# Tables by GpSimd, odd inverse decays through PSUM, earlier rows and scatter of each third chunk, and W2's first load moved to the fourth half

## The reference

```
state = 0
for t in range(768):                                   # per batch and head
    y[t]  = r[t] @ (state + outer(u * k[t], v[t]))
    state = w[t][:, None] * state + outer(k[t], v[t])
x = y as 3072 tokens x 384
h = x @ w_in;  g = max(h, 0) + alpha * min(h, 0);  x = g @ w_out       # 384 -> 2048 -> 384
expert = argmax(x @ w_gate);  gate = softmax(x @ w_gate)[expert]       # 8 experts
out = gate * (max(x @ w1[expert], 0) @ w2[expert])                     # 384 -> 1024 -> 384
```

## Time and profile before

| | us |
|---|---|
| median of 3 runs | 778.72 (777.6 to 780.84) |
| profiled execution, its own time | 781.25 |
| its span | 779.5 |
| PE busy | 733.1 (94%) |
| DVE, ACT, POOL busy | 475.7, 365.6, 392.9 |
| first output product of g = 0, 1, 2, 3, 4, 5, 6, 7 | 50.6, 122.8, 184.2, 248.4, 309.4, 370.8, 432.2, 491.0 |

### The profile page before, as it was taken

How to read it: one execution, slowest core, us unless ns; L and a number is a source line. 1 busy time by engine, 2 the same in 40 slices (tenths; PEclk the granted TensorE clock), 3 DMA queues, 4 the chain that set the end, 5 groups by cost and what they waited for, 6 DMA issues and landing times.

```text
span 779.5 us, 17757 instructions
## 1 busy us (share of the span) xinstructions
PE 733.1 (94%) x6779; PEld 516.6 (66%) x6779; DVE 475.7 (61%) x967; ACT 365.6 (47%) x735; POOL 392.9 (50%) x372
## 2 busy tenths in 40 slices
PE   4699999999989999999999999998999999999995
PEld 4466656656655665665666666556688878788783
DVE  6998898779666878776787864645333333333331
ACT  3652577656655756746756665542122212212210
POOL 5445488769668869778777876252111111111111
PEclk9998999999999999999999999999999999999998
DMA  9835636365364653645545247994699866766763
GB/s 341 324 150 185 209 132 244 105 241 174 131 238 179 234 215 121 233 165 172 201 142 187 82 162 243 341 345 158 225 383 395 294 245 214 254 237 219 265 222 116
DMA packets 42694, 170.04 MB, mean 218 GB/s; under 512 B 5198, under 2 KB 13136, under 8 KB 37104
## 3 DMA queue, kind: packets, MB, share of 16 engines
q1 hardware_dynamic: 30160, 108.18, 39.1%
q10 hardware_dynamic: 8928, 50.51, 18.5%
q0 software_dynamic: 3520, 10.17, 3.3%
HBM read 132.30 MB, written 37.33 MB: 218 GB/s over the span
## 4 chain that ended last, share of the span: by engine, by line
PE 60%; POOL 9%; DMA 9%; DVE 6%; issue 6%; ACT 3%; SPq 1%; ACTq 0%; POOLq 0%; DVEq 0%
PE bank L1733 5%; PE bank L1876 5%; PE bank L1878 5%; PE bank L1877 5%; PE bank L1735 4%; PE bank L1734 4%; PE bank L1724 4%; PE bank L1722 4%; PE bank L1721 4%; PE bank L1842 4%; PE bank L1844 4%; PE bank L1843 4%; DMA arena<-w_exp_dram 3%; POOL act_buf L606 3%; DMA route_rows<-xrow,pos 2%
## 5 line engine op out<-in xcount | busy, mean ns | idle before, releaser
L606 POOL TENSOR_TENSOR act_buf<-act_buf 128x384 f16<-128x384 f32 x128 | 120.2, 939 | 139.8 <-ACT act_buf L809 138.8
L1291 DVE SCALAR_TENSOR_TENSOR act_buf<-neg,slope,bank 128x384 f32<-128x384 f32 x128 | 77.7, 607 | 92.1 <-ACT neg L802 91.4
L692 POOL DMA_INDIRECT out_dram<-neg,dest x28 | 27.5, 984 | 201.7 <-DVE neg L1560 194.2
L1733 PE MATMUL bank<-arena,act_buf 128*128 128x392 f16 x384 | 127.2, 331 | 1.6 <-ACT xrow L765 1.4
L1721 PE MATMUL bank<-xh,arena 128*128 128x384 f16 x384 | 125.5, 327 | 2.2 <-DVE xl L1093 1.5
L1734 PE MATMUL bank<-arena,act_buf 128*128 128x392 f16 x384 | 127.1, 331 | 0.0
L1735 PE MATMUL bank<-arena,act_buf 128*128 128x392 f16 x384 | 127.0, 331 | 0.0
L1722 PE MATMUL bank<-xl,arena 128*128 128x384 f16 x384 | 125.3, 327 | 0.0
L1842 PE MATMUL bank<-shared,arena 128*128 128x128 f16 x672 | 114.1, 219 | 1.9 <-DVE shared L1486 1.7
L1844 PE MATMUL bank<-shared,arena 128*128 128x128 f16 x672 | 114.1, 219 | 0.0
L1843 PE MATMUL bank<-shared,arena 128*128 128x128 f16 x672 | 114.1, 219 | 0.0
(11 more groups left out here) (185 smaller groups left out, 1563.9 us busy)
## 6 DMA issues: line engine op xcount, KB each, us to landing
arena<-expert_split ACTq DMA_DIRECT2D x28, 1536.0 KB, 7.5
arena<-w_exp_dram SPq DMA_DIRECT2D x32, 768.0 KB, 6.3
expert_split<-arena SPq DMA_DIRECT2D x32, 768.0 KB, 4.7
arena<-expert_split SPq DMA_DIRECT2D x9, 1536.0 KB, 9.2
arena<-rk_in_dram SPq DMA_DIRECT2D x24, 512.0 KB, 6.0
arena<-rk_tok_dram SPq DMA_DIRECT2D x24, 384.0 KB, 3.3
arena<-w_dram SPq DMA_DIRECT2D x24, 256.0 KB, 6.8
shared<-route_rows ACTq DMA_DIRECT2D x31, 197.0 KB, 2.5
```

The lines of the kernel that those rows point to most:

```text
L606: pool.tensor_tensor(gl[:, f % 4, :], gf[:, f % 4, :], gh[:, f % 4, :], ALU.subtract).then_inc(gl_done, 1)
L1733: pe.matmul(at, gh[:, f % 4, ts], woh[:, f, :], start=(f == 0), stop=False)
```

## The change

Seven of the eight small table copies go from DVE's turn 13 of g = 0 to POOL's start; the eighth, of an unused tensor, goes. Where the hidden bank of the turn is free, the reciprocals are written there, multiplied from there, and copied to their place (`inverses_through`), for chunk 2 in turn 1 and chunk 1 in turn 14 of g > 0; hidden tiles 2 and 4 wait for that. `y_rows` of chunk 2 goes from turn 13, behind the product of tile 13, to turn 12. The scatters go ahead of the decayed k and q of their turn, the third from turn 15 to 14. `load_w2(0)` is issued in the middle of SP's list of g = 3.

```diff
 # SP, middle(g, j)
                 if b < B:
                     load_tok(b, half, 1)
                     load_v(b, half, 1)
+                if g == 3:
+                    sp.wait_ge(wide_free[0], 4)
+                    load_w2(0)
                 store_hu(j + 1)
                 load_hu(j + 3)
...
             for g in range(1, 2 * B - 1):
                 middle(g, FIRST_UNIT[g] // 2)
-                if g == 2:
-                    sp.wait_ge(wide_free[0], 4)
-                    load_w2(0)
 # POOL
+            pool.wait_ge(pool_const, 3)
+            pool.tensor_copy(expert_no[:, :], iota_i[:, 0:NE])
+            pool.tensor_copy(token_no[:, :], iota_i[:, 8:8 + NC])
+            pool.tensor_copy(region[:, :], iota_i[:, 16:16 + NE])
+            pool.tensor_copy(slot_no[:, :], iota_i[:, 32:32 + REST])
+            pool.tensor_copy(begin[:, :], iota_i[:, 16:16 + NE + 1])
+            pool.tensor_copy(lane[:, :], iota_i[:, 8:9])
+            pool.tensor_copy(next_row[:, :], iota_i[:, 16:16 + NE + 1]).then_inc(pool_const, 1)
...
                         if f in lows and not end:
                             unit_low(unit + lows.index(f))
+                        if not start and not end and f in (12, 13, 14):
+                            scatter(g - 1, f - 12)
                         if not last:
                             if f == 11:
                                 decayed_k(b + 1, half, 0)
...
-                        if not start and not end and f in (12, 13, 15):
-                            scatter(g - 1, (12, 13, 15).index(f))
 # DVE
+            def inverses_through(b, half, c, odd, read):
+                m, at = 6 * b + 3 * half + c, (half + c) % 2
+                dve.wait_ge(scan_done, m + 1)
+                dve.wait_ge(kt_done, m - 1)
+                dve.wait_ge(g_done, UP + read)
+                dve.reciprocal(odd.rearrange("p (a j) -> p a j", a=NP),
+                               prod[:, c, :, 1:C + 1].rearrange("p a (j r) -> p a j r", r=2)[:, :, :, 1]
+                               ).then_inc(odd_done, 1)
+                dve.wait_ge(odd_done, m + 1)
+                every_second = inv[:, at, :].rearrange("p (j r) -> p j r", r=2)
+                dve.tensor_tensor(every_second[:, :, 0], odd,
+                                  w_tile(m).rearrange("p (j r) -> p j r", r=2)[:, :, 1], ALU.mult)
+                dve.tensor_copy(every_second[:, :, 1], odd).then_inc(inv_done, 1)
...
                         if not start and f == 1:
-                            inverses(nb, nh, 2)
+                            inverses_through(nb, nh, 2, b_hid[f][:, 0:NP * C // 2], NF * g + f + 1)
...
                         if f % 4 == 1 and f > 3:
                             if update(nh, c) and nh + c > 0:
                                 decayed_state(nb, nh, c)
-                            y_rows(nb, nh, c, b_y)
+                            if f < 13:
+                                y_rows(nb, nh, c, b_y)
...
                         if f == 12:
                             decays(b + 1, half, 1, b_hid[f][:, 0:C])
+                    if not end and f == 12:
+                        y_rows(nb, nh, 2, b_y)
...
-                    if start and f == 13:
-                        dve.wait_ge(pool_const, 3)
-                        dve.tensor_copy(ident_h[:, :], ident[:, :])
-                        dve.tensor_copy(expert_no[:, :], iota_i[:, 0:NE])
-                        dve.tensor_copy(token_no[:, :], iota_i[:, 8:8 + NC])
-                        dve.tensor_copy(region[:, :], iota_i[:, 16:16 + NE])
-                        dve.tensor_copy(slot_no[:, :], iota_i[:, 32:32 + REST])
-                        dve.tensor_copy(begin[:, :], iota_i[:, 16:16 + NE + 1])
-                        dve.tensor_copy(lane[:, :], iota_i[:, 8:9])
-                        dve.tensor_copy(next_row[:, :], iota_i[:, 16:16 + NE + 1]).then_inc(dve_const, 1)
                     if not last:
-                        if f == 14:
+                        if f == 14 and start:
                             inverses(b + 1, half, 1)
+                        if f == 14 and not start:
+                            inverses_through(b + 1, half, 1, b_hid[f][:, 0:NP * C // 2], NF * g + f + 1)
 # PE, hidden(...)
+                if f == 2 and not first and not last_half:
+                    pe.wait_ge(inv_done, NC * (g + 1) + 2)
+                if f == 4 and not first and not last_half:
+                    pe.wait_ge(inv_done, NC * (g + 1) + 3)
```

More of the change, by code:

```diff
@@ L90, in build @@
         ident = sb("ident", [128, 128], F32)
-        ident_h = sb("ident_h", [128, 128], F16)
         earlier = sb("earlier", [128, C], I32)
@@ L458, in _, with load_w2 @@
             load_tok(1, 0, 2)
+            def load_w2(e):
+                for i in range(2):
+                    sp.wait_ge(split_out[i], UP + 16 * (2 * e + 2))
+                sp.dma_start(arena[:, w2_at(e):w2_at(e) + 2 * UNIT], wsplit[e][:, 2 * UNIT:4 * UNIT]
+                             ).then_inc(w2_in[e], 16)
             def middle(g, j):
@@ L1301, in mlp @@
                         if not start and f == 1:
-                            inverses(nb, nh, 2)
+                            inverses_through(nb, nh, 2, b_hid[f][:, 0:NP * C // 2],
+                                             NF * g + f + 1)
                         if f == 2:
@@ L1350, in mlp @@
                         w_out_low(1, f // 11)
-                    if start and f == 13:
-                        dve.wait_ge(pool_const, 3)
-                        dve.tensor_copy(ident_h[:, :], ident[:, :])
-                        dve.tensor_copy(expert_no[:, :], iota_i[:, 0:NE])
-                        dve.tensor_copy(token_no[:, :], iota_i[:, 8:8 + NC])
-                        dve.tensor_copy(region[:, :], iota_i[:, 16:16 + NE])
-                        dve.tensor_copy(slot_no[:, :], iota_i[:, 32:32 + REST])
-                        dve.tensor_copy(begin[:, :], iota_i[:, 16:16 + NE + 1])
-                        dve.tensor_copy(lane[:, :], iota_i[:, 8:9])
-                        dve.tensor_copy(next_row[:, :], iota_i[:, 16:16 + NE + 1]).then_inc(dve_const, 1)
                     if not last:
-                        if f == 14:
+                        if f == 14 and start:
                             inverses(b + 1, half, 1)
+                        if f == 14 and not start:
+                            inverses_through(b + 1, half, 1, b_hid[f][:, 0:NP * C // 2],
+                                             NF * g + f + 1)
                         if f == 15:
@@ L1366, in mlp @@
                     if start and f == 15:
-                        dve.wait_ge(dve_const, 3)
+                        dve.wait_ge(pool_const, 4)
                     if not start and not end:
```

## The result

The changed kernel is slower: 796.54 us median of 6 runs (791.18 to 801.52) against 776.53 for the kernel before (its three runs and three more), a ratio of 1.0252 (95% interval 1.0216 to 1.0287). The forecast was 773.0.

The account below looks back on a forecast made before the run. TensorE, busy 733.1 of 779.5 us, was taken as the bound, so only earlier starts count. Gains 5.2 + 2.5 + 0 + 0 - 2.0 = 5.7 us took the median 778.72 to 773.0, range 768.0 to 778.0.

Parts of the forecast that it names:

- Odd inverses in PSUM: Turns 1 and 14: multiply and copy take 0.84 us against 0.42 to 3.32; worth nothing, 1 us lost as other end.
- the chain above: VectorE's queue from `row_sums` of turn 15 through `v_low` to `att_l`: 1.2 us given back in g=2, 0.2 in g=4.
- the one above it: The step on tables made by POOL, which quoted a multiply with two SBUF inputs taking 0.42 us once and 3.32 elsewhere.
- Third scatter: Scatter in turn 14: ScalarE's row copy waits only for PE; row copy and `att_l` waits go, 2.5 us gained, bounds 1.5 and 2.5.
- Third y rows: `y_rows` in turn 12 ahead of product 13: 6.6 us of `ytok` waits and clock gained, 1.4 given back, net 5.2.
- The four waits: PE's waits for `ytok` in g=1, 2, 4 and 5 (1.06, 2.09, 1.19, 0.54 us), forecast to go.
- the 1.7 of clock: 1.7 us lost in g=2 to PE's lower clock level after the idle 2.09 us, counted as regained.
- W2's load: In g=3 it delays the unit conversion of turn 12 (wait about 7.6 us for 3.68); PE idles 2.0, bounds 0 and 9.
- Tables: Small copies moved from VectorE in g=0 to POOL's start: PE then waits for a DMA-bound scan; nothing, 0.4 lost to 1.6 gained.
- The waits for the inverses: PE's hidden products of tiles 2 and 4 wait for inverses made over 3 and over 1 us earlier; cost nothing.
- Rival B: POOL and VectorE behind the late unit are the bound; 1 us more given back in five halves: 777.5; chance 0.15.
- C: W2 in the full stretch of g=3 decides: 780.0 us, over 782.6 if other loads are late too; chance 0.06.

Follow-up runs that it names:

- run 1: Changed kernel with the inverse of turn 1 made in SBUF without the copy, as before: 777.84 us against 777.35, ratio 1.0001.
- run 4: Changed kernel with one wait added on POOL: the decayed k of chunk 2 in turn 1 waits for `v_low` of chunk 0: 771.86 us, ratio 0.9942.
- run 2: Kernel before with only the inverse of turn 1 through PSUM, hidden tile 4 waiting for it: 778.33 us against 777.35, ratio 1.0012.
- run 5: Kernel before with only the scatters moved (turns 12, 13, 14, ahead of the decayed q): 774.30 us against 775.59, ratio 0.9975.
- run 6: Kernel before with the scatters moved and the inverse of turn 1 through PSUM: 787.77 us, ratio 1.0168.
- run 10: Kernel before with `y_rows` of the third chunk in turn 12 and the scatters moved, every inverse in SBUF: 773.06 us, ratio 0.9965.
- run 12: Kernel before with only the tables made by POOL at the start: 776.40 us against 775.61, ratio 1.0005.
- run 8: Changed kernel with POOL's decayed k of chunk 2 waiting for `v_low` and W2's load back behind the list of g=2: 768.55 us, ratio 0.9909.
- run 3: Changed kernel with `v_low` of chunk 0 moved from turn 2 to turn 3: 791.59 us, ratio 1.0165.
- run 13: Changed kernel with a write-only POOL memset added in turn 1 before the decayed k of chunk 2: 801.39 us against 776.22, ratio 1.0321.
- run 14: Changed kernel with a POOL copy from SBUF to SBUF added in turn 1 before the decayed k of chunk 2: 801.24 us, ratio 1.0316.
- run 15: Changed kernel with W2's load behind the list of g=2 as before: 785.57 us, ratio 1.0105.

## Why the prediction was wrong

- **The step that failed** is that of *Odd inverses in PSUM*: "it is already in the chain above, and where PE doesn't wait for that chain it is worth nothing". The chain had `v_low` in it as one more item, at the lengths of before (0.55 to 1.37 in the trace), although the same step and the one above it quoted 3.32 for another instruction with two SBUF operands. The slow multiply of turn 1 was not only a cost. POOL's decayed k waits for it by semaphore, so POOL stood for some 0.4 us in most halves; the multiply got through there, and `v_low` behind the instruction that followed. Made fast, it let POOL run on, and `v_low` took over its place with a longer hold: 5.8 for 3.3. PE then waited 15.7 us for `att_l` and lost 6.0 to the clock, where the step said nothing, or 1 us at its other end. Runs 1 and 4 take the loss away from the changed kernel, runs 2, 5 and 6 build it up in the kernel before.
- *Third scatter*: right in its size alone (774.30 for 775.59; 2.5 us taken, 1.9 by the ratio). What it did besides was the second half of the loss: it removed the other pause, POOL's wait for ScalarE.
- *Third y rows*: 5.2 us taken, nothing alone and about 0.8 beyond the scatters (0.9965 for 0.9975, the intervals overlap). The four waits went as I said; the loss at the boundary was mis-sized. I had the chain to `att_l` and left the row copy out of this step, because another part of the change was to mend it: 3.23 us and its clock. Beside the scatters the row copy is no longer late, and still little is left: against run 5, run 10 waits 3.3 us less for `ytok`, 1.9 more for `att_l` and 1.6 more for the hidden product behind VectorE's. And the 1.7 of clock came from one profile; runs 5 and 12 have `ytok` as before, their longest waits for it are 1.5 us, and no lower level follows.
- *W2's load*: right in mechanism, mis-sized in time. ScalarE's wait in turn 12 of g=3 came to 8.09 us in the changed kernel against my 7.6. PE paid 1.08 and 0.80 us there, near my 2.0, if by luck in part: the wait at the next boundary, in which I had put most of it, can't be told from the hold. Alone it costs 4.7 us, since `y_rows` then stands behind it (5.70 us and 2.4 of clock).
- *Tables*: right. The wait moved to the scan behind its DMA, 0.8 us, with 1 more at `turn_k`; 1.0005.
- *The waits for the inverses* that PE got: none shows in any run.
- Rival B had the right queue, POOL's, and a price of 1 us a half in place of 4 to 7; it thought of POOL's own lateness, not of what its work does to VectorE. Only C named a time beyond 782.6, and for loads that are late, not for this. A bound for `v_low` could have been had from the trace of before: the five instructions that POOL has in line there take 0.9, 1.3, 0.9, 1.2 and 1.6 us, so up to 5.9 us a half by this estimate.

Not settled: what exactly POOL needs to hold VectorE out. In run 5 the inputs of L606 were there about 0.3 us before L557 ended and `v_low` got in; in g=3 of the changed kernel they were there 1.1 us before, and it didn't. That distance alone does not decide: at the boundary before the decayed k the inverse had been ready for 1.0 us in g=2 and in g=3 of the changed kernel, and `v_low` had begun 0.3 us behind the start of POOL's low part in both, yet it got in in g=2 alone. The cause stays open; what is shown is that without a pause of POOL the hold can last through five instructions, and with one it doesn't. Nor was it tried how much the inverse of turn 14 brings: runs 8 and 10 differ by both inverses, the added wait and the tables, 0.9909 against 0.9965, some 4.4 us, each in a group of its own.

## What to carry to other kernels

A stall can be a gap that another engine lives on: before making an instruction faster or a wait shorter, ask which queue will now run without a pause, and which instruction of the other engine will be held by it. For VectorE beside GpSimd, list every instruction with two SBUF operands and bound each by the unbroken run of GpSimd's work that can stand beside it, not by its mean length. Where one is on the path, order a pause by a semaphore; half a microsecond of it in each half was worth some 24 us here.

## What the runs showed of the hardware

- A VectorE instruction of 0.55 us with two SBUF operands was held for 5.5 to 6.2 us in 20 halves of six kernels (the changed one and runs 3, 6, 13, 14 and 15), until POOL's queue paused; a write-only memset of 0.42 us in the middle of the train didn't let it in. In other halves it got in between two POOL instructions without a pause, and the second was then 0.3 us longer (1.60 for 1.26 in g=2 of the changed kernel; 1.23 for 0.90 in run 5). VectorE operations with one operand in PSUM kept their length beside the same work (0.43, 0.41, 0.61).
- From g=1 to g=7, PE's waits of up to 1.9 us left the granted clock at 1.00. Of those of 2.1 us and more all but two (2.88 in run 3, 2.83 in run 13) were followed by some 3 to 6.3 us of PE's work at its lower level, 0.50 to 0.53. In g=0 every profile has such a stretch too, with no long wait shortly before it.
